# Turning the projection on U round: x as the stationary operand, one batch in the attention tail, the other inside the first mixer block

## The reference, cut to what matters

```python
attn_out = attention(q, k, v)                 # 2 batches, 8 heads, 768 rows, head_dim 64, local window and 8 global keys
x = attn_out as [2, 768, 512]
# second layer, the "mixer"
xt = x.transpose(0, 2, 1)
h = xt @ U @ V                                # U is 768 x 32, V is 32 x 768
u = x + h.transpose(0, 2, 1)
x = u + np.maximum(u @ w_ch1, 0.0) @ w_ch2    # 512 -> 2048 -> 512
# third layer: gate, choice of one of 8 experts per row, two matmuls per row
```

## Time and profile before

| what | value |
|---|---|
| median of three runs | 653.5 us (652.47 to 653.63) |
| the profiled execution | 656.84 us, of which the span from the first to the last instruction is 654.6 us |
| TensorE busy | 597.1 us (91% of the span) |
| TensorE weight loads busy | 522.4 us (80%) |
| VectorE, ScalarE, GpSimd busy | 271.5, 242.5, 118.0 us |
| mean granted TensorE clock | 0.958 of 2.4 GHz |

### The profile page before, as it was taken

The page is one execution under the profiler, slowest core; times in us unless marked ns, Lnnn a source line. Parts: engine busy times, 40 slices in busy tenths (PEclk is TensorE's granted clock), DMA queues, the critical chain, the costliest instruction groups (busy, mean ns, idle before and its releaser), DMA issues.

```text
span 654.6 us, 9497 instructions
## 1 busy us (share of the span) xinstructions
PE 597.1 (91%) x3238; PEld 522.4 (80%) x3239; DVE 271.5 (41%) x563; ACT 242.5 (37%) x400; POOL 118.0 (18%) x128
## 2 busy tenths in 40 slices
PE   2899998899999999999999999438799998999995
PEld 2899994698989989899989998336688786887884
DVE  5366665544331121212221112755647257475421
ACT  5688873333212011111111113306536356365321
POOL 7989820000000000000000000001111212112121
PEclk9899998899999999999999999657899998999998
DMA  7697523232110000100010000544857248574210
GB/s 271 254 324 277 192 78 128 70 127 96 66 52 29 1 1 0 50 1 0 1 47 3 0 1 1 178 144 131 282 196 230 99 142 279 191 247 163 90 43 24
DMA packets 24627, 73.78 MB, mean 113 GB/s; under 512 B 2784, under 2 KB 3312, under 8 KB 24593
## 3 DMA queue, kind: packets, MB, share of 16 engines
q1 hardware_dynamic: 21584, 65.37, 29.0%
q0 software_dynamic: 2592, 7.62, 3.6%
q10 hardware_dynamic: 416, 0.33, 0.2%
HBM read 67.02 MB, written 7.08 MB: 113 GB/s over the span
## 4 chain that ended last, share of the span: by engine, by line
PE 86%; DVE 4%; POOL 3%; DMA 2%; ACT 2%; issue 2%; POOLq 0%; DVEq 0%; ACTq 0%; SPq 0%
PE bank L456 64%; PE bank L1177 4%; PE bank L1189 3%; PE bank L1211 3%; PE bank L919 3%; PE bank L1210 2%; PE bank L500 2%; DMA raw<-in_w_dram 2%; PE bank L519 2%; ACT hs L974 1%; POOL bias L1426 1%; PE bank L528 1%; DVE wbuf L601 1%; PE bank L863 1%; POOL k_parts L1419 1%
## 5 line engine op out<-in xcount | busy, mean ns | idle before, releaser
L456 PE MATMUL bank<-uT,wbuf 128*128 128x384 f32 x768 | 144.9, 337 | 1.4 <-DVE uT L686 1.4
L456 PE MATMUL bank<-wbuf,hid 128*128 128x512 f32 x576 | 145.2, 396 | 0.0
L456 PEld LDWEIGHTS bank<-uT,wbuf 128*128 128x128 f32 x768 | 136.2, 188 | 7.1 <-DVE uT L686 1.8
L456 PEld LDWEIGHTS bank<-wbuf,hid 128*128 128x128 f32 x576 | 106.0, 188 | 20.6 <-issue 0.8
L721 DVE SCALAR_TENSOR_TENSOR hid<-bank,hid 128x384 fp32r<-128x384 f32 x64 | 35.7, 558 | 208.5 <-ACT hid L663 208.5
L663 ACT ACTIVATE hid<-bank 128x384 fp32r<-128x384 f32 x64 | 31.4, 491 | 226.3 <-PE bank L456 226.3
L456 PE MATMUL bank<-wbuf,xT 128*128 128x512 f32 x360 | 93.0, 409 | 1.7 <-DVE xT L1004 1.7
L601 DVE TENSOR_TENSOR wbuf<-raw,wbuf 128x1024 fp32r<-128x1024 f32 x64 | 75.4, 1221 | 25.9 <-ACT wbuf L597 25.7
L456 PE MATMUL bank<-wbuf,hT 128*128 128x512 f32 x360 | 85.9, 394 | 0.0
L456 PEld LDWEIGHTS bank<-wbuf,xT 128*128 128x128 f32 x360 | 69.7, 197 | 16.3 <-issue 2.1
L597 ACT CAST wbuf<-raw 128x1024 fp32r<-128x1024 f32 x64 | 64.5, 1048 | 43.9 <-DMA raw<-in_w_dram 22.2
(11 more groups left out here) (169 smaller groups left out, 563.4 us busy)
## 6 DMA issues: line engine op xcount, KB each, us to landing
raw<-in_w_dram SPq DMA_DIRECT2D x64, 512.0 KB, 4.6
raw<-in_w_ch_dram SPq DMA_DIRECT2D x16, 512.0 KB, 4.2
k_raw<-in_kT_dram SPq DMA_DIRECT2D x7, 960.0 KB, 4.9
vs<-in_vw_dram SPq DMA_DIRECT2D x8, 715.0 KB, 4.7
q_raw<-in_qT_dram SPq DMA_DIRECT2D x7, 768.0 KB, 7.6
mixed<-x SPq DMA_DIRECT2D x12, 256.0 KB, 2.1
k_raw<-in_kT_dram SPq DMA_DIRECT2D x1, 640.0 KB, 5.5
q_raw<-in_qT_dram SPq DMA_DIRECT2D x1, 512.0 KB, 6.3
```

Source lines behind the costliest of these rows:

```text
L456: last = pe.matmul(dst, lhs[a], rhs[b_], start=start and i == 0, stop=stop and i == 2)
```

## The change

The stationary side of the projection becomes a 128 x 128 piece of `x`, the moving side the 32 columns of `U`. For each batch that is 4 column pieces of `x` times 6 row tiles, 24 plain fp32 matmuls. The result is h1 transposed (512 rows in four pieces, 32 columns), so it is copied out by ScalarE three times side by side (`keep_h1T`) and transposed back by four transposes (`turn_h1`).

Batch 0's projection stands after the last scores (g = 47), its transposes an iteration later. Batch 1's stands in block 0 after step f = 13, its transposes after f = 14. The first weight entry and the high part of V are split by ScalarE during attention, their low parts by GpSimd after its last q/k split. The entries come in another order (w_ch1 and w_ch2 in turn), and steps 0 to 12 each split one. In memory a filler (`early_lows`) moves `q_parts` away from the low part of the first entries.

```diff
-        u_sb = sb("u_sb", [P, TB, 3, R])
+        u_sb = sb("u_sb", [P, TB, R])
+        sb("early_lows", [P, UNITS // 2, UNIT], F32, early)
-        ENTRIES = [(0, i) for i in range(RAW)]
-        for i in range(RAW):
-            ENTRIES += [(1, i), (0, RAW + i)]
-        ENTRIES += [(1, i) for i in range(RAW, UNITS)]
+        ENTRIES = [(which, i) for i in range(UNITS) for which in range(2)]
+        def project(pe, b):
+            pe.wait_ge(const_in, 32)
+            for c in range(DC):
+                for t in range(TB):
+                    last = pe.matmul(h1_bank(b)[0][:, c * R:(c + 1) * R], x[:, b * TB + t, c * P:(c + 1) * P], u_sb[:, t, :],
+                                     start=t == 0, stop=t == TB - 1)
+            last.then_inc(h1_done, 1)
+        def turn_h1(pe, b):
+            pe.wait_ge(h1_kept, b + 1)
+            for c in range(DC):
+                last = pe.transpose(h1_bank(b)[1][0:3 * R, c * P:(c + 1) * P], u2T[:, c * 3 * R:(c + 1) * 3 * R], ident[:, :])
+            last.then_inc(h1_turned, 1)
 mixer_pe:
-            pe.wait_ge(attn_done, 1)
-            pe.wait_ge(const_in, 32)
-            pe.wait_ge(y_out, 16)
-            for b in range(B):
-                for t in range(TB):
-                    last = pe.matmul(bank[5 + b][0:3 * R, :], u_sb[:, t, :, :].rearrange("p a r -> p (a r)"), x[:, b * TB + t, :],
-                                     start=t == 0, stop=t == TB - 1)
-                last.then_inc(h1_done, 1)
-            pe.wait_ge(h1_lo, B)
+            pe.wait_ge(v_lo, 1)
+            pe.wait_ge(h1_lo, 1)
             for j in range(BLK):
                 mix(j)
...
+                    if kb == 0 and f == NF - 3:
+                        pe.wait_ge(attn_done, 1)
+                        project(pe, 1)
+                    if kb == 0 and f == NF - 2:
+                        pe.wait_ge(u_done, TB)
+                        turn_h1(pe, 1)
+                    if kb == 1 and f == 0:
+                        pe.wait_ge(h1_lo, 2)
 entries_after:
-            if f < 2 * RAW:
-                return [RAW + 1 + f]
-            return [2 * RAW + (f + 1) // 2] if f % 2 and f < NF - 1 else []
+            return [3 + f] if 3 + f < 2 * UNITS else []
+        def h1_bank(b):
+            return (bank[0], bank[1]) if b == 0 else (bank[7], bank[5])
+        def keep_h1T(act, b):
+            act.wait_ge(h1_done, b + 1)
+            act.copy(u2T[:, 0:DC * 3 * R]..., h1_bank(b)[0][:, 0:DC * R]... .to_broadcast([P, DC, 3, R])).then_inc(h1_kept, 1)
+        def keep_h1_hi(act, b): ...      # h1_parts[:, b] <- bank, after h1_turned
+        def keep_h1_lo(dve, b): ...      # subtract, after h1_hi
 mixer_act, before the loops:
-            act.copy(v_parts[:, :], v_raw[:, :]).then_inc(v_hi, 1)
-            for k in range(RAW):
-                entry_hi(act, k)
-            (h1_parts of both batches)
+            entry_hi(act, 1)
             for j in range(BLK):
                 keep_u(j, u_event(j))
-            entry_hi(act, RAW)
+            entry_hi(act, 2)
 mixer_dve, before the loops:
-            (v_parts low, entry_lo 0 to 3, h1 low of both batches) ... entry_lo(dve, RAW)
+            (mix and keep_u of three tiles, then)
+            dve.wait_ge(lo_split, 1)
+            entry_lo(dve, 1)
+            entry_lo(dve, 2)
 attention loop on TensorE:
+                    if g == GROUPS - 1:
+                        pe.wait_ge(normed, PAIRS)
+                        pe.wait_ge(scored, 2 * (GROUPS - 1))
+                        project(pe, 0)
+                    if g == GROUPS:
+                        turn_h1(pe, 0)
 on ScalarE:
+                        if g == GROUPS - 2 * TB + 1:
+                            keep_v_hi(act)
+                        if g == GROUPS - TB + 1:
+                            entry_hi(act, 0)
+                    if g == GROUPS - 1:
+                        keep_h1T(act, 0)
+                    if g == GROUPS:
+                        keep_h1_hi(act, 0)
 on VectorE:
+                    if g == GROUPS + TURN_LAG - 1:
+                        keep_h1_lo(dve, 0)
                 normalise(PAIRS - 1, 1)
                 dve.wait_ge(normed, 2 * PAIRS)
+                dve.memset(lim[:, 6:7], 0.0).then_inc(attn_done, 1)
 on GpSimd, after the last split_qk:
+            pool.wait_ge(v_hi, 1)
+            (low part of v_parts).then_inc(v_lo, 1)
+            pool.wait_ge(v_lo, 1)
+            entry_lo(pool, 0)
```

More of the change, by code:

```diff
@@ L247, in build @@
         h1_done = sem("h1_done")
+        h1_kept = sem("h1_kept")
+        h1_turned = sem("h1_turned")
         h1_hi = sem("h1_hi")
@@ L250, in build @@
         v_hi = sem("v_hi")
+        v_lo = sem("v_lo")
         ht_done = sem("ht_done")
@@ L548, in mixer_pe @@
                 turn(j, u_event(j))
+            pe.wait_ge(y_out, 16)
             for kb in range(NB):
@@ L616, in entries_after, with keep_h1_hi, keep_h1_lo, keep_v_hi @@
         def entries_after(f):
-            if f < 2 * RAW:
-                return [RAW + 1 + f]
-            return [2 * RAW + (f + 1) // 2] if f % 2 and f < NF - 1 else []
+            return [3 + f] if 3 + f < 2 * UNITS else []
[3 more added lines that the diff above has]
+            act.wait_ge(h1_done, b + 1)
+            act.copy(u2T[:, 0:DC * 3 * R].rearrange("p (c a r) -> p c a r", c=DC, a=3),
+                     h1_bank(b)[0][:, 0:DC * R].rearrange("p (c a r) -> p c a r", c=DC, a=1).to_broadcast([P, DC, 3, R])
+                     ).then_inc(h1_kept, 1)
+        def keep_h1_hi(act, b):
+            act.wait_ge(h1_turned, b + 1)
+            act.copy(h1_parts[:, b, :], h1_bank(b)[1][0:3 * R, :]).then_inc(h1_hi, 1)
+        def keep_h1_lo(dve, b):
+            band = slice(2 * R, 3 * R)
+            dve.wait_ge(h1_hi, b + 1)
+            dve.tensor_tensor(h1_parts[band, b, :], h1_bank(b)[1][band, :], h1_parts[band, b, :].bitcast(F32),
+                              ALU.subtract).then_inc(h1_lo, 1)
+        def keep_v_hi(act):
+            act.wait_ge(const_in, 32)
+            act.copy(v_parts[:, :], v_raw[:, :]).then_inc(v_hi, 1)
         def first_expert_hi(act, i0, i1):
@@ L645, in keep_u2 @@
                 act.copy(u2T[:, :], bank[6][:, :]).then_inc(ut_act, 1)
-            act.wait_ge(const_in, 32)
-            act.copy(v_parts[:, :], v_raw[:, :]).then_inc(v_hi, 1)
-            for k in range(RAW):
-                entry_hi(act, k)
-            for b in range(B):
-                act.wait_ge(h1_done, b + 1)
-                act.copy(h1_parts[:, b, :], bank[5 + b][0:3 * R, :]).then_inc(h1_hi, 1)
+            entry_hi(act, 1)
             for j in range(BLK):
                 keep_u(j, u_event(j))
-            entry_hi(act, RAW)
+            entry_hi(act, 2)
             for kb in range(NB):
@@ L666, in mixer_act @@
                             entry_hi(act, k)
+                        if f == NF - 3:
+                            keep_h1T(act, 1)
+                        if f == NF - 1:
+                            keep_h1_hi(act, 1)
                     if (j := is_u2(kb, f)) is not None:
@@ L698, in keep_logits @@
                                 bank[7][:, 0:BLK * NG].rearrange("p (t e) -> p t e", t=BLK)).then_inc(lg_out, 1)
[L700 to L709, removed]
             for j in range(BLK):
@@ L713, in mixer_dve @@
                 keep_u(j, u_event(j))
-            entry_lo(dve, RAW)
+            dve.wait_ge(lo_split, 1)
+            entry_lo(dve, 1)
+            entry_lo(dve, 2)
             for kb in range(NB):
@@ L725, in mixer_dve @@
                             entry_lo(dve, k)
+                        if f == NF - 1:
+                            keep_h1_lo(dve, 1)
                     if f == 0 and kb:
@@ L1097, in load_consts @@
             def load_consts():
-                sp.dma_start(u_sb[:, :, :, :], moe_U).then_inc(const_in, 16)
+                sp.dma_start(u_sb[:, :, :], moe_U).then_inc(const_in, 16)
                 sp.dma_start(v_raw[:, :], moe_V).then_inc(const_in, 16)
@@ L1378, in _ @@
                         normalise(*divmod((g - TB) // HALF, 2))
+                    if g == GROUPS + TURN_LAG - 1:
+                        keep_h1_lo(dve, 0)
                 normalise(PAIRS - 1, 1)
                 dve.wait_ge(normed, 2 * PAIRS)
+                dve.memset(lim[:, 6:7], 0.0).then_inc(attn_done, 1)
             with dve.Else():
                 full_dve(dve, ng, nl)
-            dve.memset(lim[:, 6:7], 0.0).then_inc(attn_done, 1)
+                dve.memset(lim[:, 6:7], 0.0).then_inc(attn_done, 1)
+                keep_h1_lo(dve, 0)
             mixer_dve(dve)
@@ L1435, in _ @@
                     split_qk(n)
+                pool.wait_ge(parts, 3 * (PAIRS - 1))
             with pool.Else():
                 full_pool(pool)
+            band = slice(R, 2 * R)
+            pool.wait_ge(v_hi, 1)
+            pool.tensor_tensor(v_parts[band, :], v_raw[band, :], v_parts[band, :].bitcast(F32), ALU.subtract).then_inc(v_lo, 1)
+            pool.wait_ge(v_lo, 1)
```

(5 more changed lines are left out.)

## The result

The changed kernel takes 658.75 us, the median of 10 runs (655.68 to 660.28). The kernel before takes 653.57 us in as many. The ratio is 1.0072, with a 95% interval of 1.005 to 1.0094: slower by 5.2 us. The forecast was 657.5, in a range of 651.5 to 662.

The account below looks back on a forecast made before the run. The prediction took TensorE, busy 91% of the span, as the bound, with its granted clock deciding. Transition -4.8 plus block 0 +8.85 gave +4.05, so 653.5 + 4.0 = 657.5 us, range 651.5 to 662.

Parts of the forecast that it names:

- The pair's price: Both projections on TensorE: 0.110 us per narrow pair, 5.3 us for a batch, 10.6 for both.
- The upper price: Projection pairs at low clock: 0.223 us each, from the traced pairs with 42 columns.
- The full-clock sum: Transition and block 0 at 2.4 GHz throughout: -9.3 + 5.75 = -3.6 us.
- 15.2: Transition from batch 0's projection to the first `up` at full clock: 9.3 + 1.05 + 0.7 + 4.1, against 24.5 before.
- The covers: Weight-entry splits, loads and h1 copies hidden under other work in attention and block 0; taken to cost 0.
- The clock: Both projections: unmixed narrow pairs make the granted clock fall in each; chance 0.74, 657.5 us.
- The first rival: Both projections: clock stays at 1.00, sum -3.6, 649.9 us; chance 0.15.
- 4.5 was put for the low clock: Batch 0's transition: +1.9 in the projection, +1.7 in the rest of attention, +0.9 in additions and transposes.
- 3.1 was put: Batch 1 in block 0: +1.9 in the projection, 1.2 in `up` and `down` behind it; 8.85 with the 5.75.
- the rival of the pair's price: Both projections: weight loads don't overlap, a pair takes 0.19, 7.7 us more, 661 or above; chance 0.03.
- the second case: Both projections: clock stays at 1.00, 649.9 us; chance 0.15.
- the third: Clock falls in only one projection: 654.4 us with batch 0 alone, 653.0 with batch 1 alone; chance 0.08.

Follow-up runs that it names:

- batch 1 in four: Changed kernel with batch 1's 48 narrow pairs cut into four stretches of 12, behind steps 10 to 13 of block 0; 655.61 us, ratio 1.0043.
- the old side at the new places: Changed kernel's new projection places, but U stationary and 512 columns of x moving as before, no h1 transposes; 651.98 us, repeats 652.01 and 655.19.
- three copies of U: Changed kernel with U three times side by side as moving operand, 96 columns a pair instead of 32; 651.41 us, ratio 0.9967, repeat 653.33.
- the filled gap: U stationary at the new places, two of batch 1's six wide matmuls put in TensorE's idle time before the transposes; 649.97 us, repeat 651.30.

## Why the prediction was right

**The pair's price.** 0.110 us was right: 5.33 us for 48 pairs in the execution that kept the clock (batch 1 in four, batch 0's stretch), 0.111 each. The upper price, 0.22 at low clock, was right as well.

**The full-clock sum.** The -3.6 was not to be seen in the changed kernel, but the old side at the new places tests its working: -4.8 expected from the same terms, -4.94 measured. The transition took 14.48 where 15.2 less the transposes and the 0.15 gives 14.6. Block 0 took 5.11 more, where 12 wide pairs are 5.15. The covers held: no step of block 0 waits for a weight entry, and ScalarE's two extra pieces in attention cost nothing that a trace shows (A is at 98.08 before and at 98.10 in the second profile of the changed kernel, each with 3.4 us of low clock ahead of it). The way from the first addition to the first `up` is 4.04 with the old side at full clock; the prediction's pieces add up to 4.0, where it wrote 4.1.

**The clock.** This decided the sign, and it was right in mechanism: in all three profiles it fell with both batches, inside batch 0's pairs and at the very end of batch 1's. The runs with three copies of U, and with batch 1 in four, show it as the cause. One widens the pairs, the other parts them, neither takes work away, and in both the clock of the altered projections stays at 1.00. The first rival had the rule of the Trainium skill behind it (TensorE: Matmul & The Clock Gate, "HAM oscillation — how this bites in real kernels"), by which gaps without work send the clock down. The trace disagrees: the clock fell at 99.2 with no gap ahead of it (2.30 of 2.30 us busy), and 10.00 of 10.00 us were busy at 0.50.

**The sizes.** Batch 0: 4.5 was put for the low clock. By A to B it is 20.82 - 15.2 = 5.6 in one profile and 18.37 - 15.2 = 3.2 in the two others (and 16.77 - 15.2 = 1.6 in the run with batch 1 in four, whose batch 0 is the same). Batch 1: 3.1 was put, on top of 5.75; measured were 7.33 - 5.75 = 1.6. The step that was off is where the clock falls in batch 1's projection: not after 31 pairs, but at its end, so that one low stretch follows and no second.

**The median.** Between A and C the traces give +3.6, +1.2 and +1.1, the medians +5.2, the forecast's sum +4.0. Part of the difference is the kernel before's: its two profiled executions are 3.3 and 3.4 above its median of 653.57, and none of its other executions was traced. But 40 of them have their time and mean granted clock on record, and the two go together: 5.6 us for 0.010 of clock by a straight line, from which they lie 0.6 us off on average. The changed kernel's median clock is 0.009 lower, which is 5.0 us on that line; its ten executions lie 0.8 us below the line, those with three copies of U 0.8, with the old side 2.9, with the filled gap 3.8. This is an estimate, and 0.953 is just outside the 0.958 to 0.968 that the line was drawn through. It says that the 5.2 us come with low clock and not with the added work. In which part of the span most executions of the kernel before have less of it than its profiles stays open.

The forecast took the profiled execution's transition, low stretches and all, as the one to subtract from, and so may have given the change too much credit. That it came within 1.3 us is luck in part: against the traces its +4.05 was 0.4 too high once and 2.9 too high twice (batch 1 priced 1.5 too high each time, batch 0 by 1.3 in two of three), and what the traces don't show filled that up.

**Small slips.** In the rival of the pair's price, 7.7 more with the clock at full rate would be 649.9 + 7.7 = 657.6, not "661 or above with either clock". The chances by direction add up to 0.14 for the second case and 0.09 for the third, where 0.15 and 0.08 were given. Neither moves the forecast.

**What was missed.** The moves can make the low stretch ahead of block 0 longer. In the kernel before 12.25 us of wide matmuls stood ahead of the mixes and transposes. With them gone, a light piece of 9 us follows: weighing pairs, 2.4 us idle, transposes. With the old side it lost the clock in two of three profiles, with three copies of U in both, and the low stretch went on into block 0. The prediction had put 0.9 on this piece, for low transposes alone. It costs 2.4 and 3.3 us with the old side, and 2.2 and 2.3 with three copies. In the changed kernel's own profiles it is there in the first alone, for 3.4 us. In both profiles of the run that fills the idle time it is gone.

## What to carry to other kernels

Which operand is stationary decides how many columns a weight load gets. When the loads set the price, 32 moving columns cost what 96 do, and a long stretch of them can also cost the clock, for itself and for the wide work behind it. Spread such a stretch between wide work, or keep the wide form, and look at the granted clock over a stretch that is fully busy before you call it bound by work.

Moving work off a transition leaves a lighter transition. Look for work that is needed later and ready now, and put it in the idle time: here 1.7 us of it won 1.7 on the path and held the clock in both profiles.

## What the runs showed of the hardware that was not expected

Pairs of 96 and of 32 moving columns both take 0.111 to 0.112 us at 2.4 GHz. In an unbroken row of 48 pairs the clock fell inside it or right behind it all seven times with 32 columns (2.4 to 5.5 us after its start), and none of four times with 96.

Twelve transposes at low clock (112.8 to 116.1) were followed by full clock (116.4 on), with nothing else on TensorE. The Trainium skill (TensorE: Matmul & The Clock Gate, "Part 4: PE-mode transpose") says that the full clock does not engage for transposes. The rows disagree, here and at 118.4 to 121.7 of the kernel before: in the low stretch transposes were all that TensorE did, and the full clock followed. With the filled gap 12 transposes ran in 1.78 us at 1.00.

The start of attention has none, 3.4 or 6.8 us of low clock from one execution to the next of the same kernel. The three profiles of the changed kernel have one of each, with A at 96.76, 98.10 and 99.58. It is one source of the spread, which is 6.7 us over the 29 timed runs of the kernel before.
